# The turned state reading goes through another bank and is split batch by batch; the first product of the states takes its high passes first

## The chip, the cores and the metric

The kernel runs on one core of one Trainium2 chip. The metric is the device time of one execution in microseconds (us); less is better. The core has five engines with a queue of instructions each: TensorE (PE, matrix products; PEld is its loading of the stationary operand), VectorE (DVE), ScalarE (ACT), GpSimd (POOL) and SyncE (SP, which here only issues transfers). They meet at semaphores. TensorE writes to PSUM, eight banks of 128 partitions x 512 float32; everything else lives in SBUF.

## The reference

```python
# attention between tokens x (8 batches, 8 heads, 512 tokens, 64) and state (8, 8, 32, 64)
scores = scale * x @ state.T;  a  = softmax(scores);  xread = a @ state
scores2 = scale * state @ x.T; a2 = softmax(scores2); sread = a2 @ x
x = concat([xread, sread], axis=2) as rows of 512          # 8 * (512 + 32) = 4352 rows
x = ((x @ w1) * (x @ w2)) @ w3 @ w_out                     # 512 -> 1024 -> 1024 -> 512
h = x @ w_in; g = h - tanh(h); out = g @ w_out2            # 512 -> 2048 -> 512
```

All data are float32. Where precision needs it, the kernel splits an operand into a high part (fp32r) and a low part, the rest (value minus high part), and takes a product in three passes: high by high, high by low, low by high (`PASSES`, pairs of stationary and moving part).

## The kernel before

Four stages follow each other on TensorE. `stage_front` does the attention of the eight batches and, between its small steps, the product w3 @ w_out in eight rows of work (`piece(r, n)`, r = 0 to 7, four pieces of six matmuls each). Then come the products of the state rows with w1 and w2, `s1(f)` for f = 0 to 7, `stage_ys`, and for the token rows `stage_moe1` and `stage_moe2`. The change touches `stage_front` alone, all of which ends before 133 us.

In the loop over the batches e, TensorE's queue is written out by hand: `scores(e)`, `piece(e, 0)`, `sread_turn(e - 1)`, `piece(e, 1)`, `scores_turn(e)`, `a_turn(e - 1)`, `piece(e, 2)`, `a2_turn(e)`, `piece(e, 3)`, `sread(e)`. The turns are transpositions against an identity.

- `scores(e)` writes px (banks 6 and 7). ScalarE copies it to stS (`copy_st`), VectorE takes the maximum (`tokens_max`: tmax, then tbias), and `scores_turn(e)` writes the turned scores to ps (banks 4 and 5).
- From ps VectorE makes a (`rows_max`, `rows_sub`), ScalarE its exponential (`exp_a`), VectorE its sum and inverse (`rows_sum`, `rows_invert`: rinv), GpSimd scales it (`rows_scale`, ready as a_ready). `a_turn` turns it to pt (banks 2 and 3), `turn_a` on ScalarE copies it to aT.
- ScalarE makes a2 from px (`exp_a2`), `a2_turn(e)` turns it to pt, `turn_a2` copies it to a2T, and `sread(e)` multiplies it with the tokens xs into ps (bank 4).
- ScalarE scales this reading of the states into sr (`copy_sr`), and `sread_turn(e)`, one transposition, is put into ps at column 512, that is bank 5. VectorE copies it to srT (`copy_srT`), one 128x128 piece per batch. Because bank 5 is in use, `scores_turn(e)` waits for that copy (`after(pe, srT_copied, e)`).

After the last batch ScalarE and VectorE split the whole srT into srs_hi and srs_lo, four instructions of 128x256 each, and `s1(0)` waits for these four in turn. Between `sread(B-1)` and `s1(0)` TensorE does two units of another product (`values.tensor_unit`, to banks 6 and 7, then 0 and 1) with `sread_turn(B-1)` between them.

w1 and w2 come by transfers into w_raw and are split by `split_w(f)` into a ring w12 of `WRING` = 4 slots; the first four splits are done in batches 4 to 7. SyncE issues the transfers of the next batch's tokens (xT after `scores`, xs after `sread`), of w3 (after `prod_done`) and of w1 and w2 in this order per batch.

Lines: 392 and 497 split_w, 376 and 483 split_w3, 398 copy_st, 406 exp_a2, 418 exp_a, 426 turn_a, 433 copy_sr, 464 and 575 the split of srT, 504 and 506 tokens_max, 518 and 524 rows_max and rows_sub, 529 to 538 rows_sum and rows_invert, 542 copy_srT, 365 rows_scale, 610 scores, 621 scores_turn, 630 a2_turn, 639 a_turn, 651 sread, 657 sread_turn, 668 piece, 685 s1, 753 ys, 112 the units, 124 and 129 their splits.

Of the kernel before, what the change touches and what calls it, by code (L numbers as in the profile page):

```python
# [64 lines left out]
def plain(ap):  # L65

    return ap.bitcast(F32)
# [3 lines left out]
PASSES = ((0, 0), (0, 1), (1, 0))  # L71
LAST = len(PASSES) - 1
WARM = 44
WRING = 4


class Map:
# [163 lines left out]
def stage_front(nc, sem, room_a, room_b, room_c, room_o, small, w_at, x_rows, x_cols, state_cols, w1, w2, w3_cols, wo, aT, aT_at, w34,  # L241
# [26 lines left out]
    stS = room_b("stS", [P, G, S])  # L268
    a2 = stS
    a2T = room_b("a2T", [P, G, J, P])  # L270
    srT = room_b("srT", [P, Q, NSTATE])
    w3T_at[1][1] = room_b.at
    w3T = [[over(f"w3T_{n}{r}", w3T_at[r][s], [P, NF1, P]) for r in range(2)] for s, n in enumerate(("hi", "lo"))]
    w3r = [over(f"w3r{r}", w3T_at[r][1], [P, NF1, P], F32) for r in range(2)]
    srs = [over("srs_hi", w3T_at[1][1], [P, Q, NSTATE]), over("srs_lo", stS_at, [P, Q, NSTATE])]

    xT_at = room_c.at
    xT = room_c("xT", [P, Q, S])
# [23 lines left out]
    tok_max, tok_bias, tok_exp, tok_guard, tok_inv = (  # L302
        sem(n) for n in ("tok_max", "tok_bias", "tok_exp", "tok_guard", "tok_inv"))
    a2_turned, a2T_out = sem("a2_turned"), sem("a2T_out")
    sread_done, sr_copied, sr_turned, srT_copied = (sem(n) for n in ("sread_done", "sr_copied", "sr_turned", "srT_copied"))
    sr_hi, sr_lo, s1_am, s1_hi = sem("sr_hi"), sem("sr_lo"), sem("s1_am"), sem("s1_hi")
    s1_done, s1_pm, s1_lo = sem("s1_done"), sem("s1_pm"), sem("s1_lo")

# [62 lines left out]
    def scalar(act):  # L371
        def split_w3(r):
            act.wait_ge(w3_in[r % 2], 16 * (r // 2 + 1))

            after(act, prod_done, r - 1)
            act.activation(w3T[0][r % 2][:, :, :], w3r[r % 2][:, :, :], ACT.Copy).then_inc(w3_hi, 1)

        def split_wo(n):
            act.wait_ge(wo_in[n], 16)
            act.activation(wos[0][:, 2 * n:2 * n + 2, :], wor[:, 2 * n:2 * n + 2, :], ACT.Copy).then_inc(wo_hi, 1)  # L380

        def empty_prod(r):
            act.wait_ge(prod_done, r + 1)
            act.activation(w34[0][:, r, :], pz[r % 2], ACT.Copy).then_inc(prod_hi, 1)

        def split_w(f):
            if f == 0:
                for ab in range(2):
                    act.wait_ge(w_in[ab], 16 * Q)

            after(act, s1_done, f - WRING + 1)
            act.activation(w12[0][f % WRING][:, :, :, :], w_raw[:, :, :, f * P:(f + 1) * P], ACT.Copy).then_inc(w_hi, 1)

        def copy_st(e):
            act.wait_ge(scored, e + 1)

            after(act, a2_turned, 2 * e)
            act.activation(stS[:, :, :], px[:, :].rearrange("p (g s) -> p g s", g=G), ACT.Copy).then_inc(st_copied, 1)

        def exp_a2(e):  # L400
            act.wait_ge(tok_bias, e + 1)

            act.wait_ge(st_turned, e + 1)
            after(act, tok_guard, e)
            for g in range(G):
                act.activation(a2[:, g, :], px[:, g * W:(g + 1) * W], ACT.Exp, scale=SCALE, bias=tbias[:, g:g + 1],
                               accum_out=tsum[:, g:g + 1]).then_inc(tok_exp, 1)

        def turn_a2(e):

            after(act, sread_done, e)
            for g in range(G):
                act.wait_ge(a2_turned, 2 * e + g + 1)
                act.activation(a2T[:, g, :, :], pt[g].rearrange("p (j c) -> p j c", c=P), ACT.Copy).then_inc(a2T_out, 1)

        def exp_a(e):
            act.wait_ge(row_sub, e + 1)
            act.activation(a[:, :, :], a[:, :, :], ACT.Exp, scale=SCALE).then_inc(row_exp, 1)

        def turn_a(e):  # L420
            act.wait_ge(a_turned, e + 1)
            if e == 6:

                act.wait_ge(prod_done, NF1 - 1)
            for g in range(G):
                act.activation(aT[:, g, e, :], pt[g], ACT.Copy).then_inc(aT_out, 1)

        def copy_sr(e):
            act.wait_ge(sread_done, e + 1)
            act.wait_ge(tok_inv, e + 1)  # L430
            after(act, sr_turned, e)
            for g in range(G):
                act.activation(sr[:, g * D:(g + 1) * D], ps[:, g * D:(g + 1) * D], ACT.Copy, scale=tinv[:, g:g + 1]).then_inc(sr_copied, 1)

        act.dma_start(sT[:, 0:1, :, :], state_cols[:, 0:1, :, :]).then_inc(sT_in[0], 16)
        split_w3(0)
        split_wo(0)
        split_wo(1)
        split_wo(2)
        copy_st(0)  # L440
        split_wo(3)
        exp_a2(0)
        split_w3(1)
        turn_a2(0)
        exp_a(0)
        empty_prod(0)
        copy_sr(0)
        for e in range(1, B):
            copy_st(e)
            if 1 < e < NF1 - 1:  # L450
                split_w3(e + 1)
            if e >= B - WRING:
                split_w(e - B + WRING)
            exp_a2(e)
            turn_a(e - 1)
            if e == 1:
                split_w3(2)
            turn_a2(e)
            empty_prod(e)
            exp_a(e)  # L460
            copy_sr(e)
        act.wait_ge(srT_copied, B)
        for k in range(KC):
            act.activation(srs[0][:, k, :], srT[:, k, :], ACT.Copy).then_inc(sr_hi, 1)
        values.scalar_unit(act, 0, 0, pv)
        for f in range(NF1):
            act.wait_ge(s1_done, f + 1)

            after(act, s1_pm, f - 1)
            act.activation(am[:, f % 2, :], bank[4 + 2 * (f % 2)][:, 0:NSTATE], ACT.Copy).then_inc(s1_am, 1)  # L470
            act.wait_ge(s1_pm, f + 1)
            act.activation(pst[0][:, f, :], pm[:, f % 2, :], ACT.Copy).then_inc(s1_hi, 1)
            if f + WRING < NF1:
                split_w(f + WRING)
            if f == 1:
                values.scalar_unit(act, 0, 1, pz)
            if f == 2:
                turn_a(B - 1)

    def vector(dve):  # L480
# [56 lines left out]
            after(dve, a_ready, e)  # L537
            dve.reciprocal(rinv[:, :], rsum[:, :]).then_inc(row_inv, 1)

        def copy_srT(e):  # L540
            dve.wait_ge(sr_turned, e + 1)
            dve.tensor_copy(srT[:, :, e * NS:(e + 1) * NS], ps[:, W:W + P].rearrange("p (q n) -> p q n", n=NS)).then_inc(srT_copied, 1)

        split_w3(0)
        split_wo(0)
# [10 lines left out]
        rows_invert(0)  # L556
        for e in range(1, B):
            tokens_max(e)
            copy_srT(e - 1)
            if 1 < e < NF1 - 1:  # L560
                split_w3(e + 1)
            rows_max(e)
            rows_sub(e)
            tokens_invert(e)
            if e == 1:
                split_w3(2)
            if e >= B - WRING:
                split_w(e - B + WRING)
            empty_prod(e)
            rows_sum(e)  # L570
            rows_invert(e)
        copy_srT(B - 1)
        for k in range(KC):
            dve.wait_ge(sr_hi, k + 1)
            dve.tensor_tensor(srs[1][:, k, :], srT[:, k, :], plain(srs[0][:, k, :]), ALU.subtract).then_inc(sr_lo, 1)
        values.vector_unit(dve, 0, 0, pv)
        for f in range(NF1):
            dve.wait_ge(s1_am, f + 1)

            after(dve, s1_hi, f - 1)  # L580
            after(dve, s1_lo, f - 1)
            dve.tensor_tensor(pm[:, f % 2, :], am[:, f % 2, :], bank[5 + 2 * (f % 2)][:, 0:NSTATE], ALU.mult).then_inc(s1_pm, 1)
            dve.wait_ge(s1_hi, f + 1)
            if f == NF1 // 2:

                dve.wait_ge(a_turned, B)
            dve.tensor_tensor(pst[1][:, f, :], pm[:, f % 2, :], plain(pst[0][:, f, :]), ALU.subtract).then_inc(s1_lo, 1)
            if f == 1:
                values.vector_unit(dve, 0, 1, pz)
            if f + WRING < NF1:  # L590
                split_w(f + WRING)

    def tensor(pe):
# [19 lines left out]
        def scores_turn(e):  # L613
            pe.wait_ge(st_copied, e + 1)

            after(pe, row_sub, e)
            after(pe, srT_copied, e)
            for g in range(G):
                for j in range(J):
                    at = j * G * P + g * P  # L620
# [11 lines left out]

        def a_turn(e):
            pe.wait_ge(a_ready, e + 1)
            for g in range(G):

                pe.wait_ge(a2T_out, 2 * e + g + 1)
# [16 lines left out]

        def sread_turn(e):
            pe.wait_ge(sr_copied, 2 * e + 2)
            pe.transpose(ps[:, W:W + P], sr[:, :], ident[:, :]).then_inc(sr_turned, 1)

        def piece(r, n):
            if n == 0:  # L660
# [12 lines left out]
        def s1(f):  # L673
# [3 lines left out]

                pe.wait_ge(v_lo, 2)
            pe.wait_ge(w_lo, f + 1)
            for ab in range(2):  # L680
                for k in range(KC):
                    if f == 0:
                        pe.wait_ge(sr_lo, k + 1)
                    for m, (s, t) in enumerate(PASSES):
                        mm = pe.matmul(bank[4 + 2 * (f % 2) + ab][:, 0:NSTATE], w12[s][f % WRING][:, k, ab, :], srs[t][:, k, :],
                                       start=k + m == 0, stop=k == KC - 1 and m == LAST)
            mm.then_inc(s1_done, 1)

        warm()
# [22 lines left out]
        values.tensor_unit(pe, 0, 1, pz)  # L712
        for f in range(NF1):
            s1(f)
            if f == 0:
                a_turn(B - 1)

    return {"sync": sync, "gpsimd": gpsimd, "scalar": scalar, "vector": vector, "tensor": tensor,
# [630 lines left out]
```

## Time and profile before

| what | value |
|---|---|
| median of the runs | 1282.47 us (3 runs, 1282.47 to 1283.27) |
| the profiled execution | 1282.32 us, of which the span of its instructions 1280.5 us |
| mean granted clock of TensorE | 0.998 |
| busy: TensorE, VectorE, ScalarE, GpSimd | 1262.3 us (99%), 779.8 (61%), 554.5 (43%), 16.0 (1%) |
| the loop over batches 1 to 7 | 20.4 to 100.4 us, 11.48 us for each of batches 2 to 6 |
| s1(0) to the end of s1 | 105.3 to about 131.3 us |

TensorE is busy nearly all the time, so what counts is where it stands still, and at which clock it runs. Times in the rows are microseconds from the span's start.

### The profile page before, as it was taken

To read this page: it belongs to the slowest core of one execution; us is meant where nothing else is said; L and a number is where in the kernel's file an instruction comes from. 1 tells how busy PE (TensorE), PEld (TensorE's weight loads), DVE (VectorE), ACT (ScalarE), POOL (GpSimd) and SP (SyncE) were. 2 spreads that over 40 slices of the span, in tenths; PEclk is the share of its full clock that TensorE was granted. 3 is DMA by queue.
4 is the path that set the end of the run, shared out by engine and by line. 5 is a ranking of instruction groups with operands and counts; after the bars stand their busy time and mean duration, and the time that the engine had idled before them with its cause. 6 is when DMAs were issued, how large, how long until landed. Compare 5 with 4: busy or idle time off the path is not lost.

```text
span 1280.5 us, 17464 instructions
## 1 busy us (share of the span) xinstructions
PE 1262.3 (99%) x6772; PEld 1016.9 (79%) x6772; DVE 779.8 (61%) x1269; ACT 554.5 (43%) x1034; POOL 16.0 (1%) x14
## 2 busy tenths in 40 slices
PE   8999999999999999999999999999999999999998
PEld 7668877777777777788888888888888888888887
DVE  6776244433333434678767677676676776776766
ACT  6665333323333333445434444444444344444443
POOL 0110000000000000000000000000000000000000
PEclk9999999999999999999999999999999999999999
DMA  9850200000000012212100100101001001010000
GB/s 364 310 198 2 83 1 33 34 1 34 34 1 33 34 34 115 66 50 67 50 1 17 50 9 9 50 18 49 0 16 49 0 17 49 16 35 7 8 34 17
DMA packets 17326, 63.77 MB, mean 50 GB/s; under 512 B 1904, under 2 KB 3056, under 8 KB 12656
## 3 DMA queue, kind: packets, MB, share of 16 engines
q1 hardware_dynamic: 16928, 62.59, 13.6%
q8 instruction: 41, 0.67, 0.2%
q10 hardware_dynamic: 336, 0.33, 0.1%
q14 instruction: 21, 0.17, 0.0%
HBM read 45.09 MB, written 17.83 MB: 49 GB/s over the span
## 4 chain that ended last, share of the span: by engine, by line
PE 57%; DVE 0%; ACT 0%; issue 0%; DVEq 0%
PE wide L1294 29%; PE bank L1272 28%; ACT ysb L1130 0%; DVE gsp_lo L1208 0%; DVE ysb L1260 0%; DVE hw L1218 0%; DVE gb L1237 0%; DVE gb L1225 0%; ACT hw L1156 0%; ACT gsp_hi L1144 0%; ACT hq L1151 0%; DVE gb L1235 0%; DVEq L1207 0%; DVEq L1223 0%
## 5 line engine op out<-in xcount | busy, mean ns | idle before, releaser
L1151 ACT ACTIVATE hq<-bank 128x512 f32<-128x512 f32 (+1 forms) x144 | 82.8, 575 | 398.3 <-PE bank L1272 398.2
L1272 PE MATMUL bank<-ysp_lo,wi_hi 128*128 128x512 f32 (+1 forms) x576 | 217.3, 377 | 0.0
L1272 PE MATMUL bank<-ysp_hi,wi_lo 128*128 128x512 f32 (+1 forms) x576 | 217.3, 377 | 0.0
L1272 PE MATMUL bank<-ysp_hi,wi_hi 128*128 128x512 f32 (+1 forms) x576 | 217.2, 377 | 0.0
L1294 PE MATMUL wide<-wz_hi,gsp_hi 128*128 128x512 f32 x544 | 212.5, 391 | 3.4 <-DVE gsp_lo L1208 2.5
L1218 DVE TENSOR_TENSOR hw<-hw,hq 128x512 f32<-128x512 f32 (+1 forms) x144 | 95.5, 663 | 197.1 <-ACT hw L1162 196.9
L1294 PE MATMUL wide<-wz_lo,gsp_hi 128*128 128x512 f32 x544 | 211.8, 389 | 0.0
L1294 PE MATMUL wide<-wz_hi,gsp_lo 128*128 128x512 f32 x544 | 211.8, 389 | 0.0
L1272 PEld LDWEIGHTS bank<-ysp_lo,wi_hi 128*128 128x128 f32 x576 | 108.4, 188 | 20.6
L1272 PEld LDWEIGHTS bank<-ysp_hi,wi_hi 128*128 128x128 f32 x576 | 108.2, 188 | 20.6
L1272 PEld LDWEIGHTS bank<-ysp_hi,wi_lo 128*128 128x128 f32 x576 | 108.2, 188 | 19.8
L1294 PEld LDWEIGHTS wide<-wz_hi,gsp_hi 128*128 128x128 f32 x544 | 102.2, 188 | 25.6 <-DVE gsp_lo L1208 4.0
L1294 PEld LDWEIGHTS wide<-wz_hi,gsp_lo 128*128 128x128 f32 x544 | 102.2, 188 | 21.5
L1294 PEld LDWEIGHTS wide<-wz_lo,gsp_hi 128*128 128x128 f32 x544 | 102.0, 188 | 20.5
L1208 DVE TENSOR_TENSOR gsp_lo<-gb,gsp_hi 128x512 fp32r<-128x512 f32 (+1 forms) x144 | 95.5, 663 | 13.5 <-ACT gsp_hi L1144 0.5
L999 PE MATMUL wide<-psp_hi,w_hi 128*128 128x512 f32 x256 | 103.3, 403 | 0.0
L1235 DVE COPY_PREDICATED gb<-far,wide 128x512 f32<-128x512 uint8 (+1 forms) x144 | 100.8, 700 | 0.1
L999 PE MATMUL wide<-psp_hi,w_lo 128*128 128x512 f32 x256 | 100.1, 391 | 0.0
L999 PE MATMUL wide<-psp_lo,w_hi 128*128 128x512 f32 x256 | 99.6, 389 | 0.0
L1237 DVE TENSOR_TENSOR gb<-bank,gb 128x512 f32<-128x512 f32 (+1 forms) x144 | 95.3, 662 | 5.0
L1225 DVE SCALAR_TENSOR_TENSOR gb<-hw,bank 128x512 f32<-128x512 f32 (+1 forms) x144 | 93.7, 651 | 0.1
L1144 ACT ACTIVATE gsp_hi<-gb 128x512 fp32r<-128x512 f32 (+1 forms) x144 | 86.1, 598 | 3.2 <-DVE gb L1237 3.2
(123 smaller groups left out, 1779.6 us busy)
## 6 DMA issues: line engine op xcount, KB each, us to landing
xT<-in_x_cols SPq DMA_DIRECT2D x8, 1024.0 KB, 8.4
xs<-in_x_rows SPq DMA_DIRECT2D x8, 1024.0 KB, 7.0
y_dram<-ysb SPq DMA_DIRECT2D x8, 1024.0 KB, 4.2
out<-ysb SPq DMA_DIRECT2D x8, 1024.0 KB, 4.6
yr<-y_dram SPq DMA_DIRECT2D x28, 256.0 KB, 4.0
w3r<-in_w_cols SPq DMA_DIRECT2D x8, 512.0 KB, 4.4
w_raw<-in_moe_w SPq DMA_DIRECT2D x8, 512.0 KB, 9.3
wi_raw<-in_moe_w_in SPq DMA_DIRECT2D x4, 1024.0 KB, 7.0
```

The source lines that it names most:

```text
L999: mm = pe.matmul(py[c], w34[s][:, f, c * P:(c + 1) * P], psp[t][:, f % 2, :], start=f + m == 0, stop=f == NF1 - 1 and m == LAST)
L1144: act.activation(gsp[0][:, slot, 0:w], gb[:, slot % 2, 0:w], ACT.Copy).then_inc(g_hi, 1)
L1151: act.activation(hq[:, f % 2, 0:w], ph[f % 2][:, 0:w], ACT.Square).then_inc(sq_done, 1)
L1208: dve.tensor_tensor(gsp[1][:, slot, 0:w], g, plain(gsp[0][:, slot, 0:w]), ALU.subtract).then_inc(g_lo, 1)
L1218: dve.tensor_tensor(u, u, q, ALU.mult).then_inc(w2_done, 1)
L1225: dve.scalar_tensor_tensor(g, u, 1.0, h, ALU.add, ALU.mult).then_inc(near_done, 1)
L1235: dve.copy_predicated(g, far[:, f % 2, 0:w], pq[f % 2][:, 0:w]).then_inc(sel_done, 1)
L1237: dve.tensor_tensor(g, h, g, ALU.subtract).then_inc(g_done, 1)
L1272: mm = pe.matmul(ph[f % 2][:, 0:w], wi[s][c][:, f * P:(f + 1) * P], ysp[k][u][c][:, 0:w], start=c + m == 0, stop=c == KC - 1 and m == LAST)
L1294: mm = pe.matmul(po[j], gsp[s][:, f % 4, j * P:(j + 1) * P], wz[u][:, f, :], start=f + m == 0, stop=f == NF2 - 1 and m == LAST)
```

## The change

The turned reading of a batch goes to bank pt[0] instead of ps, after ScalarE has emptied pt[0] of the turned a2 (`pe.wait_ge(a2T_out, 2 * e + 1)`), and before `a_turn` of that batch writes there. It isn't copied: ScalarE takes its high part and VectorE its low part right out of the bank (`split_sr`), batch by batch, into srs_hi and srs_lo. `a_turn(e)` waits for `sr_lo`. `scores_turn` no longer waits for a copy. `s1(0)` waits for all high parts, does the passes that use only srs_hi first (16 of its 24 matmuls), and waits for the low parts then. srs_hi takes srT's room, srs_lo that of the fourth slot of the ring w12, so `WRING` becomes 3 and the first three splits of w are done in batches 5 to 7.

In the order of ScalarE `exp_a(e)` goes ahead of `empty_prod(e)`, and on VectorE `rows_sum(e)` does. For the last batch `exp_a`, `rows_sum` and `rows_invert` go behind the split of sr and the first unit's splits, `a_turn(7)` goes from behind `s1(0)` to behind `s1(2)`, and `turn_a(7)` from f = 2 to f = 3.

```diff
-WRING = 4
+WRING = 3
...
-    srT = room_b("srT", [P, Q, NSTATE])
+    srs_hi = room_b("srs_hi", [P, Q, NSTATE], F32R)
...
-    srs = [over("srs_hi", w3T_at[1][1], [P, Q, NSTATE]), over("srs_lo", stS_at, [P, Q, NSTATE])]
+    srs = [srs_hi, over("srs_lo", w_at + WRING * 2 * Q * 2 * P * 4, [P, Q, NSTATE])]
...
+        def split_sr(e):
+            act.wait_ge(sr_turned, e + 1)
+            act.activation(srs[0][:, :, e * NS:(e + 1) * NS], pt[0][:, 0:P].rearrange("p (q n) -> p q n", n=NS), ACT.Copy).then_inc(sr_hi, 1)
...
             copy_st(e)
+            split_sr(e - 1)
...
             turn_a2(e)
+            if e < B - 1:
+                exp_a(e)
             empty_prod(e)
-            exp_a(e)
             copy_sr(e)
-        act.wait_ge(srT_copied, B)
-        for k in range(KC):
-            act.activation(srs[0][:, k, :], srT[:, k, :], ACT.Copy).then_inc(sr_hi, 1)
+        split_sr(B - 1)
         values.scalar_unit(act, 0, 0, pv)
+        exp_a(B - 1)
...
-            if f == 2:
+            if f == 3:
                 turn_a(B - 1)
...
-        def copy_srT(e):
-            dve.wait_ge(sr_turned, e + 1)
-            dve.tensor_copy(srT[:, :, e * NS:(e + 1) * NS], ps[:, W:W + P].rearrange("p (q n) -> p q n", n=NS)).then_inc(srT_copied, 1)
+        def split_sr(e):
+            dve.wait_ge(sr_hi, e + 1)
+            at = slice(e * NS, (e + 1) * NS)
+            dve.tensor_tensor(srs[1][:, :, at], pt[0][:, 0:P].rearrange("p (q n) -> p q n", n=NS), plain(srs[0][:, :, at]), ALU.subtract
+                              ).then_inc(sr_lo, 1)
...
             tokens_max(e)
-            copy_srT(e - 1)
+            split_sr(e - 1)
...
+            if e < B - 1:
+                rows_sum(e)
             empty_prod(e)
-            rows_sum(e)
-            rows_invert(e)
-        copy_srT(B - 1)
-        for k in range(KC):
-            dve.wait_ge(sr_hi, k + 1)
-            dve.tensor_tensor(srs[1][:, k, :], srT[:, k, :], plain(srs[0][:, k, :]), ALU.subtract).then_inc(sr_lo, 1)
+            if e < B - 1:
+                rows_invert(e)
+        split_sr(B - 1)
         values.vector_unit(dve, 0, 0, pv)
+        rows_sum(B - 1)
+        rows_invert(B - 1)
...
             after(pe, row_sub, e)
-            after(pe, srT_copied, e)
...
         def a_turn(e):
             pe.wait_ge(a_ready, e + 1)
+            pe.wait_ge(sr_lo, e + 1)
...
             pe.wait_ge(sr_copied, 2 * e + 2)
-            pe.transpose(ps[:, W:W + P], sr[:, :], ident[:, :]).then_inc(sr_turned, 1)
+            pe.wait_ge(a2T_out, 2 * e + 1)
+            pe.transpose(pt[0][:, 0:P], sr[:, :], ident[:, :]).then_inc(sr_turned, 1)
...
+            order = [(ab, k, m) for ab in range(2) for k in range(KC) for m in range(LAST + 1)]
+            if f == 0:
+
+                pe.wait_ge(sr_hi, B)
+                order.sort(key=lambda step: PASSES[step[2]][1])
+            for at, (ab, k, m) in enumerate(order):
+                s, t = PASSES[m]
+                if f == 0 and t == 1 and PASSES[order[at - 1][2]][1] == 0:
+                    pe.wait_ge(sr_lo, B)
...
             s1(f)
-            if f == 0:
+            if f == 2:
                 a_turn(B - 1)
```

## Rows read from the trace of the kernel before

**Rows 1.** What TensorE waited for: engine, line, releaser; total us, times, longest

```profile
PE wide L621 <- DVE srT L542: 4.3, 7, 0.7
PE wide L685 <- DVE srs_lo L575: 2.5, 1, 2.5
```

**Rows 2.** Timeline of TensorE in batch 6: start us, us, what

```profile
77.49 1.09 PE L610 MATMUL wide<-xT,sT 64*32 64x512 f32 x16
...
79.78 0.39 PE L668 MATMUL bank<-wos_hi,w3T_lo 128*128 128x512 f32 x1
80.00 0.27 PE L657 MATMUL wide<-ident,sr 128*128 128x128 f32 x1
...
81.27 0.40 PE L668 MATMUL bank<-wos_hi,w3T_lo 128*128 128x512 f32 x1
82.33 1.06 PE L621 MATMUL wide<-ident,stS 128*128 128x128 f32 x8 [0.66 <-DVE srT L542]
83.22 1.04 PE L639 MATMUL wide<-ident,a 128*128 128x128 f32 x8
```

**Rows 3.** Timeline of the other engines around batch 6, idle time before in brackets

```profile
77.20 0.69 DVE L493 TENSOR_TENSOR w_lo<-bank,w_hi 128x512 fp32r<-128x512 f32 x1 [1.38 <-ACT w_hi L384]
...
78.69 1.03 ACT L398 ACTIVATE stS<-wide 128x1024 f32<-128x1024 f32 x1 [0.17 <-PE wide L610]
...
80.05 1.92 POOL L365 TENSOR_TENSOR a<-a,rinv 128x1024 f32<-128x1024 f32 x1 [9.57 <-DVE rinv L538]
...
81.08 0.91 DVE L506 TENSOR_SCALAR tbias<-tmax 128x2 f32<-128x2 f32 x1
...
81.90 0.28 DVE L542 COPY srT<-wide 128x128 f32<-128x128 f32 x1
...
83.47 0.69 ACT L406 ACTIVATE stS<-wide,tbias 128x512 f32<-128x512 f32 x1 [1.45 <-issue]
```

**Rows 4.** Durations: ns min/median/max of two lines, and a group's busy us and mean

```profile
L506 DVE TENSOR_SCALAR tbias<-tmax x8: 169/905/907, 15.3 to 92.6; 128x2 f32<-128x2 f32 x8
L575 DVE TENSOR_TENSOR srs_lo<-srT,srs_hi x4: 409/413/1643, 103.5 to 105.8; 128x256 fp32r<-128x256 f32 x4
L433 ACT ACTIVATE sr<-wide,tinv 128x64 f32<-128x64 f32 x16 | 4.1, 310 | 0.0
```

**Rows 5.** Timeline at the end of the last batch and of s1(0)

```profile
100.44 1.09 PE L112 MATMUL wide<-w_raw,sT 64*32 64x512 f32 x16
...
101.78 1.09 PE L112 MATMUL bank<-w_raw,sT 64*32 64x512 f32 x16
...
103.00 1.91 POOL L365 TENSOR_TENSOR a<-a,rinv 128x1024 f32<-128x1024 f32 x1 [9.56 <-DVE rinv L538]
...
105.33 0.40 PE L685 MATMUL wide<-srs_hi,w_hi 128*128 128x256 f32 x1 [2.46 <-DVE srs_lo L575]
...
109.53 0.28 PE L685 MATMUL wide<-srs_lo,w_hi 128*128 128x256 f32 x1
109.65 0.28 PE L685 MATMUL wide<-srs_hi,w_lo 128*128 128x256 f32 x1
```

**Rows 6.** Stretches: length, busy us (count) by engine, granted clock, DMA share, GB/s

```profile
100.44:105.33 4.89, 2.43 (x40) 0.53 (x34) 4.08 (x7) 3.26 (x9) 1.91 (x1) 1.00 0.00 0
105.33:109.77 4.44, 4.44 (x25) 4.44 (x26) 2.06 (x5) 0.06 (x1) 0.00 (x0) 0.62 0.02 4
109.77:132.31 22.54, 22.33 (x185) 21.86 (x183) 12.17 (x21) 11.30 (x24) 0.00 (x0) 1.00 0.00 1
```

**Rows 7.** Timeline of TensorE, scores_turn in batch 1

```profile
24.93 1.06 PE L621 MATMUL wide<-ident,stS 128*128 128x128 f32 x8 [0.33 <-DVE srT L542]
```

**Rows 8.** Transfers issued from 31 to 42 us: KB each, us to landing

```profile
xT<-in_x_cols SPq DMA_DIRECT2D x1, 1024.0 KB, 9.1
```

**Rows 9.** Timeline of batch 3: its scores and the split of w3

```profile
43.05 1.09 PE L610 MATMUL wide<-xT,sT 64*32 64x512 f32 x16
...
47.22 1.06 ACT L376 ACTIVATE w3T_hi<-w3r 128x1024 fp32r<-128x1024 f32 x1 [1.94 <-DMA w3r<-in_w_cols]
```

More of the change, by code:

```diff
@@ L304, in stage_front @@
     a2_turned, a2T_out = sem("a2_turned"), sem("a2T_out")
-    sread_done, sr_copied, sr_turned, srT_copied = (sem(n) for n in ("sread_done", "sr_copied", "sr_turned", "srT_copied"))
+    sread_done, sr_copied, sr_turned = (sem(n) for n in ("sread_done", "sr_copied", "sr_turned"))
     sr_hi, sr_lo, s1_am, s1_hi = sem("sr_hi"), sem("sr_lo"), sem("s1_am"), sem("s1_hi")
@@ L679, in s1 @@
             pe.wait_ge(w_lo, f + 1)
-            for ab in range(2):
-                for k in range(KC):
-                    if f == 0:
[L683 to L686, printed above, removed]
+            order = [(ab, k, m) for ab in range(2) for k in range(KC) for m in range(LAST + 1)]
[6 more added lines that the diff above has]
+                    pe.wait_ge(sr_lo, B)
+                mine = [step for step in order if step[0] == ab]
+                mm = pe.matmul(bank[4 + 2 * (f % 2) + ab][:, 0:NSTATE], w12[s][f % WRING][:, k, ab, :], srs[t][:, k, :],
+                               start=(ab, k, m) == mine[0], stop=(ab, k, m) == mine[-1])
             mm.then_inc(s1_done, 1)
@@ L714, in tensor @@
             s1(f)
-            if f == 0:
+            if f == 2:
                 a_turn(B - 1)
```

## The prediction

> **What bounds the kernel now.** I read these views in this order. The busy shares come first: TensorE works 99% of the span (the table above). So an edit gains only where TensorE stands still or runs at a lower clock. The list of what TensorE waits for is short: seven waits before scores_turn, 4.3 us together, for the copy srT, and one of 2.5 us before the first s1 product [rows 1]. The diff touches both. All of it lies in the first 132 us; from the product ys on the work is the same and is carried over unchanged.
>
> Write T for the start of scores(e). In batch 6 T is 77.49 [rows 2]. The last product before scores_turn starts at 81.27, scores_turn at 82.33, although its input stS was copied at T+2.2 (78.69 + 1.03). The other engines show why [rows 3]: the copy srT starts at 81.90 and ends at 82.18, 0.15 before scores_turn. It is queued behind tbias, which runs 81.08 to 81.99 and ends when GpSimd's scaling does (80.05 + 1.92 = 81.97). That is a lock and not work: the same instruction takes 0.169 us at its shortest and 0.905 at the median [rows 4].
>
> At the end of the last batch [rows 5] the second unit starts at 101.78 and s1(0) at 105.33. Between them lie the copy srT, ScalarE's four high parts and VectorE's four low parts. The first low part again waits out GpSimd (busy 103.00 to 104.91): 1.643 us against 0.413 at the median [rows 4]. After this idle stretch TensorE is granted 0.62 over s1(0), a mix of its levels 2.4 and 1.2 GHz, where the stretch before had 1.00 [rows 6]: s1(0) takes 4.44 us.
>
> **The change, part by part.**
>
> *Turned reading into bank pt[0], no copy srT.* scores_turn(e) loses its wait. It can then follow the last product of piece(e,1) as sread_turn does, whose matmul stands 0.22 after the one before it (79.78 to 80.00), or at most 0.30. It starts 1.06 after it now, so 0.76 to 0.84 is gained; the bare wait in the list, 0.66, is the lower bound. I take 0.79 for batches 2 to 7. Batch 1 waits 0.33 where the others wait 0.66 [rows 7], so 0.79 − 0.33 = 0.46. Sum 6 × 0.79 + 0.46 = 5.2 us (bounds 4.3 and 5.5).
>
> What is late next after each of these? I go through the batch with scores_turn at T+4.05 instead of T+4.84.
>
> a_turn(e−1) now waits for sr_lo as well as for GpSimd's a. By its own queue it comes 0.89 after scores_turn (82.33 to 83.22), at T+4.94. GpSimd ends at T+4.48. The new low part on VectorE stands where the copy did: T+4.41 to T+4.69. Its price lies between the copy's 0.28 and the 0.41 of a subtraction twice as wide [rows 4]; I take 0.30, being near the copy, and a_turn is free at T+4.9. It just fits. It has more room from batch 2 on, because rows_sum now comes ahead of empty_prod: rows_invert moves forward by about 0.5 us, and with it GpSimd and the end of tbias.
>
> The Trainium skill (SBUF — State Buffer, "Who interferes with whom") says that a VectorE instruction with two SBUF inputs, or in a two-port mode, is fully blocked by a GpSimd instruction that reads SBUF, and that one with at most one SBUF input outside these modes is not. The trace agrees for the first half: tbias and the first low part end just after GpSimd. By the second half the new low part, one input of which is in PSUM, could even run beside GpSimd; my sum doesn't need it.
>
> ScalarE gets one more instruction a batch: the high part, 128x128, between copy_st and the split of w3. sr_turned comes at 80.00 + 0.27, T+2.8, so ScalarE ends it near T+3.2 (0.31 for 128x64 [rows 4], so about 0.3 to 0.4). The splits of w3 and w then end at T+5.2 in batches 5 and 6; with three ring slots batch 4 has no split of w. exp_a2 could start 1.14 after scores_turn (82.33 to 83.47), at T+5.19, and ScalarE has 1.45 us of idle before it now [rows 3]. Scores_turn eats 0.79 of that, the high part and its wait the rest. Nothing lost, within 0.1. From exp_a2 on the old sequence holds: a2_turn follows scores_turn at the same distance.
>
> exp_a ahead of empty_prod: ScalarE then empties the product some 0.3 us later, and nothing on TensorE needs it for another batch. copy_sr no longer has exp_a before it in the last batch. rows_max stays at T+5.9 or earlier, its result is due at sread (T+9.7). VectorE is idle 1.38 us before it takes the product now [rows 3]; 0.8 of that goes. Cost nothing; if this cover were gone, each tenth would cost 0.1 × 7.
>
> Transfers don't get faster. xT is issued at T+1.2 and needs up to 9.1 us [rows 8], so it lands at T+10.3; a batch now lasts 11.48 (43.05 to 77.49 is three of them [rows 2, 9]) and would last 10.69. That fits by 0.4 in batch 2. The split of w3 in batch 3 waits for its transfer until 47.22, T+4.2 [rows 9], and stands ahead of exp_a2 on ScalarE: it would end at T+5.2, on the edge, and a little more overlap with the transfer of w makes it late. I charge 0.4 us in all for batches 2 to 4 (bounds 0 and 1.5).
>
> Loop: 5.2 − 0.4 = 4.8 us.
>
> *End of the last batch.* Four high parts, four low parts and a copy give way to one of each, right behind the transposition. A unit's 16 matmuls take 1.09, so s1(0) could start 1.0 to 1.1 after 101.78; I take 102.80. Is its input there? sread_turn would run at 101.5 in the old frame, ScalarE's part ends about 0.6 later (102.1 to 102.2), before 102.8; the wait for sr_lo comes only after the 16 high matmuls of s1(0), and VectorE's part is done by 102.6. GpSimd is idle then, since exp_a, rows_sum and rows_invert of the last batch now come behind. So the wait goes whole: 105.33 − 102.80 = 2.5 us.
>
> *Clock.* With no idle stretch s1(0) should run at the level of the stretch before: 24 matmuls × 0.12 (109.53 to 109.65) = 2.9 us for 4.44, 1.55 gained (bounds 0 and 1.7; the latter is 0.38 × 4.44).
>
> *Rest of s1.* The stretch from 109.77 to 132.31 lasts 22.54 us [rows 6]. Work in it: 7 × 24 × 0.12 = 20.16, the turn of a 0.79 (eight transpositions), six first matmuls of ys 0.72, together 21.67. 0.87 are small waits, about 0.4 of them before ys, for the last pm; the others come from VectorE being behind with the products pm. With a_turn after s1(2) instead of s1(0), and turn_a after f = 3, I laid ScalarE's and VectorE's queues out again with the measured lengths: s1(f) is never held by pm or by the split of w, the nearest is s1(7), by 0.3 us. A ring of three slots brings one more split of w into this stretch, 1.05 + 1.2 us, in f = 0, when both engines are idle. Gain 0.3 (bounds −0.3 and 0.5).
>
> *Sum:* 4.8 + 2.5 + 1.55 + 0.3 = 9.2 us. The profiled execution took 1282.32 (span 1280.5 and 1.8 around it), so 1273.1. The median of the runs is 1282.47, 0.15 more, which changes nothing.
>
> **The rivals.**
>
> *The clock falls anyway (0.12).* From the end of the last piece to s1(0) TensorE has 3.3 us of sread, units and a transposition, all small matmuls. Against it: between 100.44 and 105.33 it had the same kinds plus 2.5 us of idleness, at a granted 1.00 [rows 6]. Price 1.5: 1274.6. The Trainium skill (TensorE: Matmul & The Clock Gate, "Part 4: PE-mode transpose") says that transpositions don't count as busy for the clock; with one of 0.3 us here it would support this rival only weakly.
>
> *Transfers bind in batches 2 to 4 (0.08).* xT or w3 land 0.5 us late in each: 1.5 instead of 0.4, 1274.2 or up to 1275.
>
> *A new wait takes the place of the old (0.05).* a_turn on sr_lo, or exp_a2 on a ScalarE that is not free, holds TensorE 0.7 in each of six batches: the loop gives 0.6 and the end stays, 1277.3. For it: margins of 0.1 in both places. Against it: they fit by the rows, and the reorder widens the first.
>
> *Slower (0.02).* The place is the low part in front of a_turn. If VectorE's subtraction is held behind something as the first one was (1.64 instead of 0.30), sr_lo comes 1.3 us late in seven batches, 9 us, and the gain is gone: 1282.3. Held over 1.7 us it decides: 1285.5 for 1.8. Against it: VectorE comes to it only when GpSimd is done.
>
> *It doesn't do what it says (0.03).* Something else releases scores_turn right behind the copy, and s1(0) is held by w or by GpSimd's part: within 0.2% of before. Against it: stS, row_sub and w are ready at least 0.8 us earlier in all these rows.
>
> **How the numbers follow.** The likeliest case has 0.70: 1273.1, on its own 1272.2 to 1274.4. Low end of the range: all terms at their best, 5.5 + 2.5 + 1.7 + 0.5 = 10.2, 1272.1, and 0.3 for what I can't see: 1271.8. High end: it takes in the clock and the transfers together (2.6 more, 1275.8) and goes on towards the new wait: 1276.8. What is left out holds some 1 to 2 in 10. Faster means under 1279.9; 0.2% is what a measurement of this kernel can tell from no change. All cases but the last two are faster: 0.95; same 0.03, slower 0.02.
>
> **What the profile after would show.** TensorE's list without srT and without srs_lo; scores_turn some 0.25 after the last product; batches of 10.7 us; ScalarE's high part of 0.3 at T+2.9 and VectorE's low part before a_turn; s1(0) at about 97.6 with a granted 1.00 and 2.9 us long; the end of s1 some 9 us earlier, and all that follows shifted alike. Wrong it would be if batches stayed near 11.4 with another name in the list (sr_lo, stS by L406, DMA), or if the clock row at s1(0) read 0.6 again.

## The result and the profile after

The changed kernel takes 1272.86 us (median of 4 runs, 1271.93 to 1273.0) where the kernel before takes 1282.87 beside it: a ratio of 0.992, 95% interval 0.9903 to 0.9937. The prediction was 1273.1 us. The profiled execution took 1272.98 us, of which the span 1271.2; before it was 1282.32 and 1280.5, so the span is 9.3 us shorter.

What TensorE waits for in the first 135 us, in the kernel after (engine, line, releaser; total us, times, longest). It answers to [rows 1]:

```profile
PE wide L606 <- POOL ident L360: 1.5, 1, 1.5
PE wide L628 <- ACT stS L398: 1.2, 1, 1.2
PE wide L637 <- ACT stS L406: 0.4, 1, 0.4
PE wide L637 <- ACT aT L426: 0.3, 1, 0.3
PE wide L767 <- DVE pm L590: 0.2, 1, 0.2
```

Both waits of [rows 1] are gone. One has come in: 0.3 us for aT, once. All the others were there before.

Timeline of the changed kernel in batch 6, T = 74.37 (L666 is sread_turn, L628 scores_turn, L647 a_turn, L548 the low part). It answers to [rows 2, 3]:

```profile
74.37 1.09 PE L618 MATMUL wide<-xT,sT 64*32 64x512 f32 x16
...
76.11 1.92 POOL L365 TENSOR_TENSOR a<-a,rinv 128x1024 f32<-128x1024 f32 x1 [8.71 <-DVE rinv L543]
...
77.19 0.28 ACT L437 ACTIVATE srs_hi<-wide 128x128 fp32r<-128x128 f32 x1 [0.60 <-PE wide L666]
...
77.88 0.18 DVE L511 TENSOR_SCALAR tbias<-tmax 128x2 f32<-128x2 f32 x1
...
77.97 0.28 DVE L548 TENSOR_TENSOR srs_lo<-wide,srs_hi 128x128 fp32r<-128x128 f32 x1
...
78.14 0.40 PE L677 MATMUL bank<-wos_hi,w3T_lo 128*128 128x512 f32 x1
...
78.31 1.05 ACT L392 ACTIVATE w_hi<-w_raw 128x1024 fp32r<-128x1024 f32 x1
...
78.38 1.04 PE L628 MATMUL wide<-ident,stS 128*128 128x128 f32 x8
...
79.26 1.04 PE L647 MATMUL wide<-ident,a 128*128 128x128 f32 x8
...
79.51 0.69 ACT L406 ACTIVATE stS<-wide,tbias 128x512 f32<-128x512 f32 x1
```

scores_turn stands 0.24 behind the last product instead of 1.06 (78.14 to 78.38), at T+4.01. GpSimd starts at T+1.74 instead of T+2.56, so tbias runs free (0.18 us) and the low part is done at T+3.9, 1.0 us before a_turn. ScalarE's queue is full: exp_a2 follows the split of w with no idle time, 1.13 behind scores_turn, which is when it may start.

Stretches of the changed kernel, from the first unit to s1(0), s1(0), and the rest until ys (length, busy us and count by engine, granted clock, DMA share, GB/s). They answer to [rows 6]:

```profile
95.64:97.94 2.30, 2.30 (x40) 0.50 (x34) 0.81 (x3) 1.43 (x5) 0.00 (x0) 1.00 0.00 0
97.94:100.92 2.98, 2.98 (x33) 2.98 (x26) 2.77 (x5) 1.28 (x2) 0.00 (x0) 1.00 0.02 5
100.92:123.03 22.11, 21.90 (x185) 21.70 (x183) 13.96 (x23) 12.25 (x25) 1.91 (x1) 1.00 0.01 1
```

The same stretches took 4.89, 4.44 and 22.54 us. These and the loop make up the whole difference: 2.59 + 1.46 + 0.43 here; 5.20 in the loop from T(1) to the first unit (80.00 us before, 74.80 after); and 0.40 is lost ahead of T(1), which lies at 20.84 instead of 20.44 because TensorE's warming transpositions took longer (the first product starts at 9.27 instead of 8.84). 5.20 + 2.59 + 1.46 + 0.43 − 0.40 = 9.28. The later stages keep their length (1148.2 us from the product ys to the end of the span in both).

One batch is longer than the others. Batches start at 31.48, 42.12, 53.10 and 63.74, so batch 3 takes 10.98 where the others take 10.64. Timeline of the changed kernel in batch 3, T = 42.12:

```profile
46.13 1.04 PE L628 MATMUL wide<-ident,stS 128*128 128x128 f32 x8
...
46.66 1.06 ACT L376 ACTIVATE w3T_hi<-w3r 128x1024 fp32r<-128x1024 f32 x1 [1.45 <-DMA w3r<-in_w_cols]
...
47.62 0.67 ACT L406 ACTIVATE stS<-wide,tbias 128x512 f32<-128x512 f32 x1
...
48.95 1.08 ACT L426 ACTIVATE aT<-wide 128x512 f32<-128x512 f32 x2
...
49.69 1.06 PE L637 MATMUL wide<-ident,stS 128*128 128x128 f32 x8 [0.26 <-ACT aT L426]
```

w3 lands at T+4.5, ScalarE's split of it ends at 47.7, and exp_a2 starts 1.49 behind scores_turn instead of 1.13. Everything behind it on ScalarE is 0.35 late, and a2_turn, which waits for aT, shows it. This is how [rows 9] go on when the batch is shorter.

### The profile page after: what moved, and what is told of

It reads as the page before. It is cut to its first block, busy times and chain, and to the rows that moved or that the text cites. A ratio compares the mean times of both kernels' runs of the same rounds, so it can differ in the third digit from the quotient of the medians.

```text
span 1271.2 us, 17472 instructions
## 1 busy us (share of the span) xinstructions
PE 1259.5 (99%) x6772; PEld 1016.3 (80%) x6772; DVE 774.1 (61%) x1265; ACT 555.0 (44%) x1038; POOL 16.0 (1%) x14
## 4 chain that ended last, share of the span: by engine, by line
PE 57%; DVE 0%; ACT 0%; issue 0%; DVEq 0%
PE wide L1308 29%; PE bank L1286 28%; ACT ysb L1144 0%; DVE gsp_lo L1222 0%; DVE ysb L1274 0%; DVE gb L1251 0%; DVE hw L1232 0%; DVE gb L1239 0%; ACT gsp_hi L1158 0%; ACT hw L1170 0%; ACT hq L1165 0%; DVE gb L1249 0%; DVEq L1221 0%; DVEq L1237 0%
```

## The experiments

All times are medians. Beside each group of experiments the kernel before ran on the same chip, with medians of 1282.3 to 1282.5 us. "T(1) to the unit" is the length of batches 1 to 7 in the profile: 80.00 us before, 74.80 after.

The medians of the kernel before hide two groups. Of its 31 executions beside the experiments, 11 took 1280.69 to 1281.05 us at a mean granted clock of 1.000, and 20 took 1282.17 to 1283.47 at 0.997 to 0.999; none lies between. The medians of the groups, 1280.9 and 1282.5, are 1.6 us apart, about what s1(0) lost to the clock in the profiled execution (1.46 us, mean clock 0.998). So it seems that the clock falls there in about two executions of three and not in the others; only an execution of the larger group has a trace. The four executions of the first comparison, 1282.47 to 1283.41, lie in the larger group.

**Only the bank.** The kernel before, with the bank and the waits of the change, and nothing else:

```diff
-            pe.transpose(ps[:, W:W + P], sr[:, :], ident[:, :]).then_inc(sr_turned, 1)
+            pe.wait_ge(a2T_out, 2 * e + 1)
+            pe.transpose(pt[0][:, 0:P], sr[:, :], ident[:, :]).then_inc(sr_turned, 1)
...
             pe.wait_ge(a_ready, e + 1)
+            pe.wait_ge(srT_copied, e + 1)
...
-            after(pe, srT_copied, e)
...
-            dve.tensor_copy(srT[:, :, e * NS:(e + 1) * NS], ps[:, W:W + P].rearrange(
+            dve.tensor_copy(srT[:, :, e * NS:(e + 1) * NS], pt[0][:, 0:P].rearrange(
```

> The kernel before with one part of the change: the turned reading goes to bank pt[0], VectorE still copies it to srT from there, a_turn waits for this copy, scores_turn for none. My theory: the loop alone gives 5.2 us (0.84 in each of batches 2 to 7, less about 0.3 for the transfer of w3 in batch 3, 0.5 in batch 1), and the end of the last batch stays as before (2.5 us of idle before s1(0), granted clock near 0.62 there): 1282.9 - 5.2 = 1277.6. Rival: without the new order on ScalarE and VectorE a_turn waits for the copy, 0.5 or more in each batch, and the gain is under 2 us.

Measured: 1276.1 us (1275.25 to 1277.75), ratio 0.9951 (0.9938 to 0.9965). The gain of the medians is 6.2 us, more than the 5.2 expected and more than the loop can give. The profiled execution was the slowest of the five, at a mean granted clock of 0.999; the other four took 1275.25 to 1276.25 at 1.000, so the fall of the clock seems to be absent in them. Like against like it is 1282.32 − 1277.75 = 4.6 us for the two profiled executions, and 1280.9 − 1275.8 = 5.1 for the medians of those at 1.000. The profile shows 4.37 in the loop (T(1) at 20.25, the first unit at 95.88, 75.63 us); the stretches behind it are those of before to 0.01 us:

```profile
95.88:100.77 4.89, 2.43 (x39) 0.53 (x34) 4.09 (x7) 3.26 (x9) 1.91 (x1) 1.00 0.00 0
100.77:105.21 4.44, 4.44 (x25) 4.44 (x25) 2.06 (x5) 0.07 (x1) 0.00 (x0) 0.62 0.02 4
105.21:127.76 22.55, 22.34 (x185) 21.87 (x183) 12.18 (x21) 11.31 (x24) 0.00 (x0) 1.00 0.00 1
```

Undisturbed batches take 10.64 here too, with the old order of exp_a and rows_sum. a_turn doesn't wait for the copy: in batch 6 it starts 0.87 behind scores_turn (78.60 to 79.47), and the copy ends at 79.28. So the rival is out. Two batches are longer, by two different transfers. Timeline of this kernel, the start of batch 4 and a2_turn in it:

```profile
52.66 1.09 PE L610 MATMUL wide<-xT,sT 64*32 64x512 f32 x16 [0.41 <-DMA xT<-in_x_cols]
...
60.53 1.06 PE L629 MATMUL wide<-ident,stS 128*128 128x128 f32 x8 [0.54 <-ACT aT L426]
```

So the bank alone is worth 5.5 in the loop, less what transfers take back (1.17 in this profile), and nothing at the end.

**Fill the idle stretch.** The kernel before, with transpositions in front of s1(0) whose results nobody reads:

```diff
         values.tensor_unit(pe, 0, 1, pz)
+        for n in range(23):
+            pe.transpose(ps[:, 0:P], ident[:, :], ident[:, :])
```

> The kernel before, with 23 transpositions of the identity to the free part of bank 4 in front of s1(0), about 2.4 us at the 0.106 us of one: they fill the idle stretch and compute nothing that is used. My theory: the low clock in s1(0) follows from the idleness, transpositions count as work, so s1(0) starts when it did and takes 3.0 instead of 4.44: 1.5 us less than before, 1281.4, granted clock 1.00. Rival (transpositions don't count for the clock): s1(0) is granted 0.6 as before, no gain.

Measured: 1280.98 us (1280.88 to 1281.47), ratio 0.9993 (0.9984 to 1.0002), an interval that takes in no change, because both groups of the kernel before are in it. The eleven executions of this kernel lie together, next to the smaller group (1280.69 to 1281.05), and none lies in the larger one. Stretches of this kernel, the filled one, s1(0), the rest:

```profile
101.86:105.49 3.63, 3.63 (x41) 2.79 (x40) 3.08 (x6) 2.31 (x6) 1.92 (x1) 1.00 0.02 5
105.49:108.50 3.01, 3.01 (x28) 3.01 (x27) 1.99 (x5) 0.00 (x0) 0.00 (x0) 1.00 0.00 0
108.50:130.97 22.47, 22.25 (x184) 21.79 (x182) 12.18 (x21) 11.31 (x24) 0.00 (x0) 1.00 0.00 1
```

s1(0) starts as late as before (4.97 us behind the first unit, 4.89 before) and takes 3.01 us instead of 4.44 at a granted 1.00. The 1.4 us are the clock's and separate from the 2.5 us of the wait. Transpositions were enough to keep the clock up, in the profile and, by their times, in all eleven executions. The rule on transpositions that the prediction names beside its first rival isn't borne out here.

**Low part behind the split of w3**, in the changed kernel:

```diff
             tokens_max(e)
-            split_sr(e - 1)
             if 1 < e < NF1 - 1:
                 split_w3(e + 1)
+            split_sr(e - 1)
             rows_max(e)
```

> The changed kernel, with VectorE's low part behind the split of w3 instead of ahead of it. This measures the margin of a_turn. My theory: a_turn then waits for sr_lo, 0.8 us in batches 2, 5 and 6 and about 2 in 3 and 4, where w3's transfer is late: 6.5 to 8.5 us slower than the changed kernel, 1280. Rival (something else sets a_turn, with slack behind it): under 2 us slower.

Measured: 1275.9 us (1275.61 to 1279.04), 3.4 above the changed kernel's 1272.5 (from the last group of runs, on another chip), not 6.5 to 8.5. Timeline in batch 6, T = 76.51:

```profile
80.52 1.03 PE L628 MATMUL wide<-ident,stS 128*128 128x128 f32 x8
...
80.59 1.23 DVE L488 TENSOR_TENSOR w3T_lo<-w3r,w3T_hi 128x1024 fp32r<-128x1024 f32 x1 [0.39 <-ACT w3T_hi L376]
...
81.73 0.29 DVE L548 TENSOR_TENSOR srs_lo<-wide,srs_hi 128x128 fp32r<-128x128 f32 x1
...
82.12 1.06 PE L647 MATMUL wide<-ident,a 128*128 128x128 f32 x8 [0.57 <-issue]
```

a_turn starts 1.60 behind scores_turn instead of 0.88: 0.72 late. The mechanism is as expected, and so is its place; it comes in batches 2 to 6, and these batches last 11.3 (one of them 11.56). The expectation failed where it added it to the lateness of w3 in batches 3 and 4: with batches 0.65 longer w3 comes in time, and ScalarE splits it at 45.37 in batch 3 (T+3.0), without waiting. In batch 4 the split comes at T+3.25 (56.91), a quarter of a us later, and that is the batch of 11.56. Otherwise the wait on the path covered the late transfer.

**a_turn(7) behind s1(0)** in the changed kernel (`if f == 2` back to `if f == 0` in TensorE's loop):

> The changed kernel with a_turn(7) behind s1(0) again, exp_a(7) and rows_sum(7) staying late. My theory: a is ready at about 103.1 only and s1(0) ends at 100.9, so TensorE stands still 2.2 us, and the clock falls after it as before s1(0) in the kernel before: 2.2 to 3.8 us slower, 1275 to 1276.7. Rival: a little idleness there is made up by waits that vanish later, under 0.5 us.

Measured: 1276.49 us (1275.41 to 1276.99). From the first unit to ys it takes 30.18 us (96.30 to 126.48) where the changed kernel takes 27.39, 2.8 more; the rest of the difference is in the loop, where batch 4 lost 1.3 to a late transfer (aT came 1.19 late). Timeline and stretches of this kernel:

```profile
103.78 1.09 PE L647 MATMUL wide<-ident,a 128*128 128x128 f32 x8 [2.05 <-POOL a L365]
```

```profile
100.90:103.78 2.88, 0.83 (x7) 0.63 (x7) 1.88 (x5) 1.52 (x3) 1.91 (x1) 1.00 0.00 0
103.78:107.00 3.22, 3.22 (x28) 3.22 (x29) 1.45 (x2) 0.23 (x1) 0.00 (x0) 1.00 0.00 0
```

So with exp_a(7) late, an early a_turn(7) costs 2.8 us. The reverse doesn't hold: with exp_a(7) early and a_turn(7) late nothing is lost (the experiment on exp_a(7) below). Both in their old places wasn't run. The clock didn't fall after this idle stretch in the profile, though I had expected it; the four executions have mean clocks of 1.000, 1.000, 0.999 and 0.998, and the two without a trace at 0.999 and 0.998 leave open whether it did there.

**Passes of s1(0) in the old order** in the changed kernel (no sorting, one wait for `sr_lo` at its start):

> The changed kernel with the passes of s1(0) in the old order, all waiting for sr_lo first. My theory: the low part is written at 97.6 and s1(0) starts at 97.9, so the new order of the passes hides nothing: the same time within 0.1 us in the trace. Rival (the order is what removes the wait): s1(0) starts 0.3 to 2 us later.

Measured: 1272.21 us (1272.04 to 1272.78). First unit at 95.41, ys at 122.80: 27.39 us, the changed kernel's own length. The new order of the passes does nothing here, since the low part is written before s1(0) starts.

**Product first in the loop** (empty_prod ahead of exp_a and rows_sum again, for batches 1 to 6):

> The changed kernel with empty_prod ahead of exp_a and of rows_sum again in the loop (last batch as changed). My theory: GpSimd ends 0.8 us later in the batch, tbias with it, the low part ends at T+4.7 and a_turn can start at T+4.83; by its queue it comes at T+4.89. It fits by less than 0.1: batches still of 10.64, no change of the total beyond 0.5 us. Rival: the margin is gone, a_turn waits 0.1 to 0.3 for sr_lo in each batch, 1 to 2 us slower.

Measured: 1272.52 us (1272.34 to 1273.35). Timeline in batch 6, T = 73.69:

```profile
76.24 1.92 POOL L365 TENSOR_TENSOR a<-a,rinv 128x1024 f32<-128x1024 f32 x1 [8.78 <-DVE rinv L543]
...
77.27 0.91 DVE L511 TENSOR_SCALAR tbias<-tmax 128x2 f32<-128x2 f32 x1
...
77.70 1.04 PE L627 MATMUL wide<-ident,stS 128*128 128x128 f32 x8
...
78.10 0.28 DVE L548 TENSOR_TENSOR srs_lo<-wide,srs_hi 128x128 fp32r<-128x128 f32 x1
```

tbias is held by GpSimd again (0.91), the low part is done at T+4.69, and a_turn starts 0.87 behind scores_turn, at 78.57, unheld, 0.19 behind the end of the low part (78.38). Where a_turn did wait for the low part it started 0.10 behind its end (82.02 to 82.12 above), so 0.1 us is left. The reorder in the loop gives a margin of 0.8 us and no time.

**exp_a(7) early.** exp_a, rows_sum and rows_invert of the last batch in the loop's order:

> The changed kernel with exp_a(7), rows_sum(7) and rows_invert(7) in the loop's order again, so ahead of the split of the last reading. My theory: ScalarE has room for exp_a(7) before the last product is done; VectorE's low part comes at T+12.8 instead of T+12.3 and s1(0) at T+12.9: 0 to 0.2 us slower. Rival (what keeps GpSimd out of the way is the late order): the low part is held until GpSimd ends, s1(0)'s last passes wait up to 0.5 and the first unit's low parts come late: 1 us or more.

Measured: 1272.28 us (1272.02 to 1274.17). First unit at 96.84, ys at 124.23: 27.39 us again. s1(0) starts 2.30 behind the unit, as in the changed kernel, and the low part isn't held: it takes 0.29 us from 98.54, while GpSimd works from 98.59 to 100.51. The profiled execution was 1.2 longer than the changed kernel's in its span, and the loop shows where. Timeline, T(3) and a2_turn of batch 3:

```profile
42.55 1.09 PE L612 MATMUL wide<-xT,sT 64*32 64x512 f32 x16 [0.56 <-DMA xT<-in_x_cols]
...
50.86 1.06 PE L631 MATMUL wide<-ident,stS 128*128 128x128 f32 x8 [1.00 <-ACT aT L426]
```

**Low part ahead of tokens_max**, so that it runs while GpSimd works:

> The changed kernel with VectorE's low part ahead of tokens_max, so that it runs while GpSimd scales a. It has one operand in PSUM and one in SBUF. My theory: it is not held by GpSimd and takes 0.28 us; tbias comes 0.4 us later in the batch, still before exp_a2 needs it: no change of the total. Rival (any subtraction is held): it lasts 0.6 us or more, until GpSimd ends, tbias at T+5.2, and each batch is 0.1 to 0.5 longer.

Measured: 1272.56 us (1272.04 to 1273.06). The low part (ns min/median/max):

```profile
L548 DVE TENSOR_TENSOR srs_lo<-wide,srs_hi x8: 291/292/294, 23.6 to 97.4; 128x128 fp32r<-128x128 f32 x8
```

In batch 6 it starts at 77.23 and GpSimd works from 75.84 to 77.76. It isn't held: a subtraction with one operand in PSUM and one in SBUF runs beside GpSimd, as the Trainium skill says (SBUF — State Buffer, "Who interferes with whom"). With both in SBUF it was held in [rows 4].

**Transfers of w1 and w2 placed otherwise** in the changed kernel, where batches 1, 2 and 3 issue 2 of them each. First 2, 0, 2, 2 over batches 1 to 4:

```diff
-            if e < Q:
-                load_w(sp, e)
+            if e in (1, 3, 4):
+                load_w(sp, {1: 1, 3: 2, 4: 3}[e])
```

> The changed kernel with the transfers of w1 and w2 for q = 2 and 3 issued in batches 3 and 4 instead of 2 and 3. Each profile of a kernel with the short batches so far lost 0 to 1.6 us in batches 2 to 4, to xT or w3 landing late. My theory: these transfers compete with w's (10 to 12 us to landing); with none of w issued in batch 2 the transfers of batch 3 land in time, T(2) to T(4) is 21.3 us without a wait, and batch 4 may lose up to 0.4: total 0.3 to 0.8 under the changed kernel run beside it, about the most that 0.06% can show. Rival (the lateness is chance of the memory and not w's load): the same waits of 0.3 to 1 us, no gain.

Then 2, 1, 1, 2:

```diff
+            for q, only in {1: [(1, (0, 1))], 2: [(2, (0,))], 3: [(2, (1,))], 4: [(3, (0, 1))]}.get(e, []):
+                load_w(sp, q, only)
```

> The changed kernel with the same six transfers of w1 and w2 spread as 2, 1, 1, 2 over batches 1 to 4 (it was 2, 2, 2, 0). Batches 2 and 3 then move 3.0 MB instead of 3.5 in 10.64 us. My theory: xT lands in under 9.3 us after its issue at T+1.2 in all batches, w3 in time, no wait of TensorE in batches 1 to 4; total 0.3 to 0.8 us under the changed kernel run beside it. Rival: as for the other placing, no gain.

And the changed kernel once more:

> The changed kernel once more, unchanged, beside the two placings of the transfers of w. It shows how far its time and its waits for xT and w3 wander: I expect 1272 to 1273.5 us and a loss of 0.3 to 1 us in batches 2 to 4 in the profile.

Measured, all beside each other: 1272.96 us (1272.27 to 1273.39), 1272.56 (1272.18 to 1273.8), and 1272.52 (1272.17 to 1272.58) for the changed kernel, which is as good as either. T(1) to the unit: 75.07, 74.95, 74.46. The two placings move the loss and don't remove it: batches 2 and 3 are free of it in both, but with two transfers of w in batch 4 it comes in batches 4 and 5. The first placing loses 0.37 and 0.24 there (52.34, 63.35, 74.23), the second 0.5 in batch 5 (62.83 to 73.97, 11.14 us), of which this is the row:

```profile
70.55 1.07 PE L638 MATMUL wide<-ident,stS 128*128 128x128 f32 x8 [0.41 <-ACT aT L427]
```

The changed kernel itself lost nothing this time: all its batches lie between 10.62 and 10.65. xT of batch 3 landed 7.1 us after its issue in it, where it took 8.9 in its first profile, with nothing changed. So the lateness wanders by itself. That it follows the transfers of w to where they are put speaks for my theory of the cause, in one profile each. One profile speaks against it as the only cause: with the low part ahead of tokens_max, batch 6 took 10.96, since scores(7) waited 0.25 for an xT that took 9.7 us to land, and none of w was under way then. The gain that I expected isn't there, and what makes the lateness wander stays open.

## Why the prediction was right

**scores_turn's wait: right, a little better than taken.** It follows the product at 0.24, so a batch gives 11.48 − 10.64 = 0.84, the upper end of what the prediction had (0.76 to 0.84; 0.79 taken), and batch 1 gives 11.13 − 10.64 = 0.49 for 0.46.

**The transfers: the right place and size for this profile, but it wanders.** I charged 0.4 for batches 2 to 4; the profile lost 0.34, to w3 in batch 3. Against the undisturbed 74.46 us of seven batches, the nine profiles with all of the short batches lost 0.34, 0.0, 1.17, 0.43, 0.03, 1.74, 0.81, 1.26 and 0.61 (the changed kernel twice, then bank only, old passes, product first, exp_a(7) early, low part ahead, a_turn(7) early, w later), and the tenth, the second placing of w, 0.49. Not all of it came in batches 2 to 4: batch 5 lost time with either placing of w, and batch 6 with the low part ahead. The bounds of 0 and 1.5 were a little too narrow at the upper end. The rival "transfers bind" came true in three of ten, so 0.08 was too little for it; its price was about right.

**What is late next: a_turn and exp_a2 fit, as worked out.** The low part took 0.28 for the 0.30 taken. That the reorder isn't needed for a_turn was foreseen, and both kernels without it (only the bank, product first) have a_turn unheld with some 0.1 to spare. No new wait in the loop other than the transfers'.

**End of the last batch: 2.59 for 2.5.** The unit, the turn and the second unit follow each other without a gap, and s1(0) comes 1.02 behind 96.92. The later place of exp_a(7) made no part of it: with exp_a(7) early the same stretch has the same length. Nor does the low part need GpSimd idle, as the prediction had it here: it ran beside it, unheld.

**Clock: 1.46 for 1.55, with some luck.** The filled kernel separates this term from the wait. But the term is there only in executions in which the clock falls, two of three by their times. The prediction took it as given because its one profile of the kernel before had it. The time of the changed kernel doesn't hang on this: from an execution of 1280.9 us, without the term, the sum leads to 1280.9 − 7.65 = 1273.2. The gain does: the changed kernel's 1272.5 to 1272.9 are some 10 us under the larger group and some 8 under the smaller. The prediction's first rival, that the clock falls anyway, didn't show: the granted clock over s1(0) was 1.00 in the profile, and the nine executions of the changed kernel lie within 1.1 us.

**Rest of s1: 0.43 for 0.3.** Before, four products of s1 came 0.1 us late (at 119.49, 122.36, 122.59 and 125.58, each 0.22 to 0.23 behind the one before it instead of 0.12); after, none does, and the wait before ys stays. That accounts for the 0.43. That they had been held by pm is the prediction's reading; no run changes this part alone.

**Not foreseen: 0.4 us ahead of T(1).** T(1) lay between 20.25 and 20.84 over the thirteen profiles of this study; the two compared here had 20.44 and 20.84. It goes with when the 44 warming transpositions at the start take up their faster pace (they start some 0.18 us apart and end at about 0.11): in the stretch from 6 to 7 us nine of them ran before, seven after, and eleven in the kernel with only the bank, which had 20.25. Without it the terms add up to 9.7 against the 9.2 of the sum. The right total owes some 0.4 us to it.

The medians moved by 10.0 us (1282.87 to 1272.86), the two profiled executions by 9.34; that difference is within the spread of single runs, 1.1 us.

## What to carry to other kernels

Before crediting the removal of a wait, walk through the same step with the new start time and name each thing that the waiter's successors need; here the prediction found three that fitted by 0.1 us or less. Two did (a_turn on the low part, exp_a2 on ScalarE), the third, w3 in batch 3, came late, and knowing them told the gain to 0.05 us a batch. When a loop with transfers behind it gets shorter, its transfers become a random wait; count it with bounds, and don't simply add it to other waits of the same batch, since they can cover each other. An idle stretch ahead of a dense stretch of products can cost more than its own length: here 2.5 us of waiting and 1.4 more at a granted 0.62. Such a fall need not come in every execution, so look at the single times, and not at their median and one profile alone, before it goes into a sum.

## What the runs showed that I had not expected

TensorE stood still 2.46 us in front of s1(0) in the kernel before and in the one with only the bank, and in both profiles the granted clock over s1(0) was 0.62. It stood still 2.05 us in front of a_turn(7) in another kernel and was granted 1.00 throughout in its profile. The fall doesn't come at a fixed place either. Timelines of the kernel with only the bank and, behind them, of the kernel before (whose first product is in [rows 5], at 105.33):

```profile
101.56 0.33 PE L686 MATMUL wide<-srs_hi,w_hi 128*128 128x256 f32 x1
101.68 0.41 PE L686 MATMUL wide<-srs_lo,w_hi 128*128 128x256 f32 x1
101.89 0.42 PE L686 MATMUL wide<-srs_hi,w_lo 128*128 128x256 f32 x1
```

```profile
105.53 0.42 PE L685 MATMUL wide<-srs_lo,w_hi 128*128 128x256 f32 x1
105.74 0.42 PE L685 MATMUL wide<-srs_hi,w_lo 128*128 128x256 f32 x1
```

With only the bank the matmuls of s1(0) begin at full pace and slow from 0.12 to 0.21 us apart at 101.7, about 0.9 us behind the restart. In the kernel before they are 0.21 apart from the second on: the granted clock is 1.00 from 105.33 to 105.50 and 0.50 from 105.6, so it fell some 0.2 us behind the restart. In both it read 1.00 while TensorE stood still, so the fall shows in the work behind the idleness. And by the times of its 31 executions the kernel before has the fall in some and not in others. So the idle stretch seems to be needed for it here (filled, it didn't come in eleven executions), but it doesn't bring it each time, and what decides isn't shown.
